# 128 unused bytes a partition ahead of the arena of a transfer-bound attention and mixture-of-experts kernel

## The chip, the cores and the metric

The kernel runs on one core of a Trainium2 chip. The metric is the device time of one execution in microseconds (us), as the median of several executions. The kernel before takes 172.38 us (three executions, 172.25 to 172.53).

## The reference

Everything is float32. Linear attention over 8 batches, 8 heads, 576 positions and 64 channels feeds a soft mixture of 8 experts:

```
kv = einsum('bhsd,bhse->bhde', k, v);  out = einsum('bhsd,bhde->bhse', q, kv)
out = out / sqrt(mean(out*out, -1) + 1e-6) * g_norm
x = out.transpose(0, 2, 1, 3).reshape(4608, 512)
logits = x @ phi                                  # (4608, 32)
d = exp(logits - logits.max(0)); d /= d.sum(0) + 1e-9
slot_input = (d.T @ x).reshape(8, 4, 512)
slot_out[e] = maximum(slot_input[e] @ w1[e], 0) @ w2[e]      # w1 (8, 512, 1024), w2 (8, 1024, 512)
c = exp(logits - logits.max(1)); c /= c.sum(1) + 1e-9
y = c @ slot_out                                  # (4608, 512)
```

## The kernel before, in words

**Memory.** One large tile, `arena`, takes 576 bytes of head (`HEAD` = 144 floats: phi, the norm's gains, and padding) and 160 blocks of 1,024 bytes in each of the 128 partitions. Loads and stores have fixed homes in it, by tables of block numbers (`KV_AT`, `Q_AT`, `W_AT`, `OUT_AT`). `place(at, n)` turns a block number into an access: n floats from 576 + 1,024 * at bytes behind the arena's start. A home is used for attention inputs first, for expert weights later, and for output rows at the end. One weight matrix, ("w1", 7), goes to the tile `xall` instead.

**Addresses.** Tiles are laid one behind another in the order in which the program makes them, each rounded up to a multiple of 32 bytes. The small working tiles of the dictionary `WORK` come first (a name has a number of buffers and a number of floats), then `arena`, `xall` and the constants. Ahead of `WORK` lie 1,152 bytes (1,024 of scratch for the DMA queue of GpSimd and four constants). The buffers of `WORK` take 18,368 bytes, so the arena begins at byte 19,520 of each partition, block 0 of the homes at 20,096, and `xall` at 183,936. 152 bytes a partition are free at the end.

**Work and order.** For each batch, K and V are multiplied into small matrices (`Kv`), whose transposes and products with phi fill `bd`. `products(T)` multiplies a tile of 128 tokens of q by `bd`, which gives attention outputs and raw logits at once. Squares, a row mean, a root and scalings give x and logits, with running sums for the slot inputs. Then 8 experts are computed from the weights as they arrive (`expert_h`, `expert_y`), and `output` makes 12 chunks of the result and stores them. The order is written out by hand. A class `Order` records every instruction, finds what it depends on, and adds the waits, so nearly every instruction is emitted by one line and the profile shows them all as L215.

**Transfers.** Each load is one DMA on SyncE's queue over 128 partitions, one contiguous row of 9,792 to 55,296 bytes in each. Five loads are issued at once, three after batch 0, and the later ones in the order of the program when their homes are free (`loads_behind`, `load_w`). The output is stored in 10 DMAs, two of them on GpSimd's queue, as 608 rows of 6,144 to 24,576 bytes; the last four chunks go as one DMA of 128 rows of 24,576 bytes. In the DMA's access every row starts at an offset that is a multiple of 1,024 bytes from block 0, at the start of `xall`, or, for the very first load (`in_first`, rows of 9,792 bytes), at the start of the arena.

Of the kernel before, what the change touches and what calls it, by code (L numbers as in the profile page):

```python
# [63 lines left out]
HEAD = 144  # L64
SCRATCH = 1024
WORK = {
    "kvT": (1, 256), "sq": (2, 1024), "part": (3, 512), "top": (1, 128), "ms": (3, 16), "r0": (2, 16), "r": (3, 16), "r1": (2, 16),
    "d": (2, 192), "alpha": (2, 1), "cm": (2, 13), "cs": (2, 13),
}
EPS_RMS = 1e-6  # L70
EPS_SUM = 1e-9
# [1052 lines left out]
```

How the kernel before makes its waits and increments, by code:

```python
    def emit(self):  # L204
        nc = self.nc
        counters = {e: nc.alloc_semaphore(f"done_{e}") for e in ENGINES[:4]}
        sems = list(counters.values())
        counts = dict.fromkeys(counters, 0)
        for op in self.ops:
            method, args, kwargs = op.call
            engine = getattr(nc, op.engine)
            *before, last = sorted(op.waits, key=lambda w: w.i) or [None]
            for w in before:
                engine.wait_ge(w.sem, w.value)
            inst = getattr(engine, method)(*args, **kwargs)
            if last is not None:
                inst.wait_op(last.sem, last.value, "sem-ge")
            if op.dma:
                op.sem, op.value = nc.alloc_semaphore(f"dma_{op.i}"), 16
                sems.append(op.sem)
                inst.then_inc(op.sem, 16)
            elif op.signals:
                counts[op.engine] += 1
                op.sem, op.value = counters[op.engine], counts[op.engine]
                inst.then_inc(op.sem, 1)
        *stores, last = [op.sem for op in self.ops if op.dma and not op.signals]
        numbers = sorted(s.num for s in sems)
        assert numbers == list(range(numbers[0], numbers[-1] + 1)) and numbers[-1] == last.num
        for sem in stores:
            nc.sync.wait_ge(sem, 16)
        nc.sync.sem_clear(range(numbers[0], last.num))
        nc.sync.wait_ge(last, 16)
        nc.sync.sem_clear(range(last.num, last.num + 1))
```

## Time and profile before

| | |
|---|---|
| median of three executions | 172.38 us (172.25 to 172.53) |
| the profiled execution's own time | 172.46 us |
| its span, first to last instruction | 171.1 us |
| granted TensorE clock, mean | 0.979 |
| moved by DMA | 71.65 MB, mean 419 GB/s over the span |
| busy: TensorE, ScalarE, VectorE, GpSimd | 148.7, 88.6, 86.5, 59.7 us |

A packet in the views of DMA is one row of a transfer, as the numbers of packets and their bytes show, or a few bytes that signal its end. The DMA share of a stretch is the time that its packets took over 16 engines' time in it; packets are counted where they start, so a short stretch can show over 100%.

### The profile page before, as it was taken

How to read it: one execution, taken by the hardware profiler on the slowest of the kernel's cores; microseconds unless marked ns; L12 is line 12 of the kernel's file. 1: busy time of each engine (PE TensorE's matmuls, PEld its weight loads, DVE VectorE, ACT ScalarE, POOL GpSimd, SP SyncE). 2: the span in 40 equal slices, each digit the busy share in tenths (PEclk: the TensorE clock that was granted, in tenths of full speed). 3: DMA queues.
4: the chain of work that ended last, by engine and by line, in shares of the span. 5: the costliest groups of instructions: out<-in, count | busy, mean ns of one | idle time of the engine just before them, and what ended most of it. 6: DMA issues, size and time to landing. Idle time of an engine off the chain costs nothing.

```text
span 171.1 us, 4194 instructions
## 1 busy us (share of the span) xinstructions
PE 148.7 (87%) x1815; PEld 102.2 (60%) x1815; DVE 86.5 (51%) x183; ACT 88.6 (52%) x230; POOL 59.7 (35%) x73
## 2 busy tenths in 40 slices
PE   7988998999999899999899998689999689989200
PEld 3457987979688787797696672256665333545000
DVE  1111437743677364763936799525887036318300
ACT  2015768786965887668849866113212044418300
POOL 7000347757356665356482589300000004000000
PEclk9999999999999999999999999999999999999965
DMA  5999999999999999899999999999999999999996
GB/s 183 435 463 396 485 405 429 434 421 483 414 409 433 443 465 427 375 431 425 421 433 444 419 412 416 440 427 408 429 425 433 462 414 398 424 428 429 422 445 264
DMA packets 3933, 71.65 MB, mean 419 GB/s; under 512 B 742, under 2 KB 742, under 8 KB 874
## 3 DMA queue, kind: packets, MB, share of 16 engines
q1 hardware_dynamic: 3562, 71.18, 97.6%
q8 instruction: 14, 0.23, 0.5%
q0 software_dynamic: 352, 0.20, 0.4%
q14 instruction: 5, 0.04, 0.1%
HBM read 61.94 MB, written 9.44 MB: 417 GB/s over the span
## 4 chain that ended last, share of the span: by engine, by line
DMA 38%; PE 35%; ACT 10%; DVE 9%; issue 1%; SPq 0%
PE psum L215 35%; DMA arena<-in_t_dram 21%; DMA arena<-in_w_dram 11%; DMA arena<-in_kv_dram 6%; DVE ms L215 3%; ACT sq L215 3%; ACT bd L215 2%; DVE logits L215 2%; ACT xall L215 1%; DVE part L215 1%; ACT arena L215 1%; ACT part L215 1%; DVE r L215 1%; ACT r L215 1%; DVE acc L215 1%
## 5 line engine op out<-in xcount | busy, mean ns | idle before, releaser
L215 PE MATMUL psum<-bd,arena 128*128 128x192 f32 (+1 forms) x320 | 56.5, 336 | 2.6 <-ACT bd L215 1.2
L215 PEld LDWEIGHTS psum<-bd,arena 128*128 128x128 f32 (+1 forms) x320 | 45.5, 179 | 10.1 <-ACT xall L215 3.5
L215 DVE TENSOR_REDUCE ms<-sq 128x16 f32<-128x1024 f32 (+1 forms) x19 | 22.0, 1162 | 28.9 <-ACT sq L215 28.8
L215 POOL TENSOR_TENSOR part<-part,r 128x512 f32<-128x512 f32 x17 | 17.8, 1049 | 49.2 <-DVE r L215 49.2
L215 POOL TENSOR_TENSOR xall<-xall,r 128x512 f32<-128x512 f32 x34 | 34.8, 1045 | 0.0
L215 ACT ACTIVATE sq<-psum 128x512 f32<-128x512 f32 x36 | 21.5, 597 | 10.7 <-PE psum L215 10.6
L215 PEld LDWEIGHTS psum<-arena 128*64 128x64 f32 (+1 forms) x640 | 18.7, 137 | 7.1 <-issue 3.2
L215 PE MATMUL psum<-arena 128*64 128x64 f32 (+1 forms) x640 | 21.3, 226 | 0.6 <-DMA arena<-in_kv_dram 0.4
L215 ACT COPY xall<-psum 128x512 f32<-128x512 f32 x34 | 20.6, 607 | 0.0
L215 ACT COPY part<-psum 128x256 f32<-128x256 f32 (+1 forms) x38 | 13.7, 360 | 10.5 <-DVE part L215 9.3
L215 DVE TENSOR_REDUCE logits<-part 128x64 f32<-128x512 f32 x17 | 17.7, 1043 | 0.0
L215 PE MATMUL psum<-arena,xall 128*32 128x256 f32 x256 | 15.0, 380 | 1.7 <-DMA arena<-in_w_dram 1.7
L215 DVE COPY arena<-psum 128x768 f32<-128x768 f32 (+1 forms) x12 | 10.5, 890 | 6.8 <-PE psum L215 6.8
L215 ACT COPY arena<-psum 128x768 f32<-128x768 f32 (+1 forms) x14 | 10.2, 754 | 7.1 <-PE psum L215 7.1
L215 PE MATMUL psum<-logits,part 32*128 32x384 f32 x96 | 12.7, 527 | 0.6 <-ACT arena L215 0.4
L215 POOL DMA_DIRECT2D out_dram<-arena x2 | 1.2, 590 | 34.2 <-DVE arena L215 34.2
L215 PEld LDWEIGHTS psum<-arena,xall 128*32 128x32 f32 x256 | 8.1, 110 | 8.2 <-issue 2.7
L215 PE MATMUL psum<-arena,sq 128*32 128x256 f32 x224 | 12.7, 379 | 0.2 <-DVE sq L215 0.2
L215 PE MATMUL psum<-xall,d 128*32 128x258 f32 x144 | 10.8, 390 | 1.2 <-ACT d L215 1.2
L215 ACT COPY bd<-psum 64x128 f32<-64x128 f32 (+1 forms) x32 | 9.9, 308 | 2.4 <-PE psum L215 2.2
L215 PEld LDWEIGHTS psum<-arena,sq 128*32 128x32 f32 x224 | 7.2, 110 | 5.1 <-DVE sq L215 0.5
L215 ACT COPY kvT<-psum 128x256 f32<-128x256 f32 (+1 forms) x9 | 3.1, 349 | 12.6 <-PE psum L215 12.6
(81 smaller groups left out, 124.9 us busy)
## 6 DMA issues: line engine op xcount, KB each, us to landing
arena<-in_w_dram SPq DMA_DIRECT2D x4, 4096.0 KB, 24.1
arena<-in_w_dram SPq DMA_DIRECT2D x4, 2048.0 KB, 21.7
arena<-in_t_dram SPq DMA_DIRECT2D x1, 6912.0 KB, 35.9
arena<-in_w_dram SPq DMA_DIRECT2D x2, 3072.0 KB, 23.2
arena<-in_kv_dram SPq DMA_DIRECT2D x2, 2304.0 KB, 19.2
arena<-in_kv_dram SPq DMA_DIRECT2D x1, 4608.0 KB, 40.5
arena<-in_kv_dram SPq DMA_DIRECT2D x1, 3584.0 KB, 30.0
arena<-in_kv_dram SPq DMA_DIRECT2D x1, 3328.0 KB, 26.0
```

What stands on the lines that cost most here:

```text
L215: inst = getattr(engine, method)(*args, **kwargs)
```

## The change

`top` moves behind `r1` in the dictionary that lays out the working tiles, and a tile `spare` of 32 floats that nothing reads or writes comes behind it. `ms`, `r0`, `r` and `r1` begin 512 bytes lower than before and `top` 640 bytes higher. All that comes after `spare`, from `d` on, begins 128 bytes higher: the arena at 19,648, block 0 of the homes at 20,224, `xall` at 184,064. 24 bytes a partition stay free. No instruction, transfer, size, order or wait is changed.

```diff
 WORK = {
-    "kvT": (1, 256), "sq": (2, 1024), "part": (3, 512), "top": (1, 128), "ms": (3, 16), "r0": (2, 16), "r": (3, 16), "r1": (2, 16),
-    "d": (2, 192), "alpha": (2, 1), "cm": (2, 13), "cs": (2, 13),
+    "kvT": (1, 256), "sq": (2, 1024), "part": (3, 512), "ms": (3, 16), "r0": (2, 16), "r": (3, 16), "r1": (2, 16),
+    "top": (1, 128), "spare": (1, 32), "d": (2, 192), "alpha": (2, 1), "cm": (2, 13), "cs": (2, 13),
 }
```

## Rows read from the trace of the kernel before

**Rows 1.** The page: busy tenths of DMA in 40 slices, packets, queues.

```profile
DMA  5999999999999999899999999999999999999996
DMA packets 3933, 71.65 MB, mean 419 GB/s; under 512 B 742, under 2 KB 742, under 8 KB 874
q1 hardware_dynamic: 3562, 71.18, 97.6%
q8 instruction: 14, 0.23, 0.5%
q0 software_dynamic: 352, 0.20, 0.4%
q14 instruction: 5, 0.04, 0.1%
```

**Rows 2.** Busy time by stretch: length, engines, granted clock, DMA share, GB/s.

```profile
0.00:5.00 5.00, 3.94 (x8) 1.70 (x9) 0.73 (x3) 1.28 (x1) 3.02 (x14) 1.00 0.61 219
5.00:165.00 160.00, 144.80 (x1809) 100.54 (x1807) 85.78 (x180) 87.35 (x229) 56.68 (x59) 1.00 1.01 429
165.00:168.50 3.50, 0.00 (x0) 0.00 (x0) 0.00 (x0) 0.00 (x0) 0.00 (x0) 0.50 0.98 421
168.50:171.10 2.60, 0.00 (x0) 0.00 (x0) 0.00 (x0) 0.00 (x0) 0.00 (x0) 0.50 0.40 170
```

**Rows 3.** The chain that ended last, in order of time: start, length, what.

```profile
34.59 35.93 DMA arena<-in_t_dram
...
116.57 18.73 DMA arena<-in_w_dram
...
135.43 1.97 PE psum L215 x32
...
159.58 0.54 DVE arena L215
```

**Rows 4.** DMA issues: size of each, us from issue to landing.

```profile
out_dram<-arena SPq DMA_DIRECT2D x1, 3072.0 KB, 10.9
...
arena<-in_first_dram SPq DMA_DIRECT2D x1, 1224.0 KB, 5.3
```

**Rows 5.** DMA from 3.96 to 4.74 us: rows of the first load alone.

```profile
DMA packets 35, 0.34 MB, mean 439 GB/s; under 512 B 0, under 2 KB 0, under 8 KB 0
q1 hardware_dynamic: 35, 0.34, 103.3%
```

**Rows 6.** DMA from 6.5 to 10 us: rows of 17,408 bytes.

```profile
DMA packets 83, 1.44 MB, mean 413 GB/s; under 512 B 0, under 2 KB 0, under 8 KB 0
q1 hardware_dynamic: 83, 1.44, 96.1%
```

**Rows 7.** DMA from 60 to 65 us: rows of 55,296 bytes.

```profile
DMA packets 41, 2.27 MB, mean 453 GB/s; under 512 B 0, under 2 KB 0, under 8 KB 0
q1 hardware_dynamic: 41, 2.27, 104.8%
```

**Rows 8.** DMA from 164 to 168.5 us: stored rows of 24,576 bytes.

```profile
DMA packets 77, 1.89 MB, mean 421 GB/s; under 512 B 0, under 2 KB 0, under 8 KB 0
q1 hardware_dynamic: 77, 1.89, 97.6%
```

**Rows 9.** DMA from 136 to 141 us: weight rows of 32,768 bytes.

```profile
DMA packets 65, 2.13 MB, mean 426 GB/s; under 512 B 0, under 2 KB 0, under 8 KB 0
q1 hardware_dynamic: 65, 2.13, 98.9%
```

**Rows 10.** Waits of TensorE: engine, for whom, us in total, times, longest.

```profile
PE psum L215 <- DMA arena<-in_w_dram: 1.7, 1, 1.7
PE psum L215 <- DVE top L215: 1.5, 2, 1.0
```

## The prediction

> **What bounds the kernel now.** I read the slices of the page first. The DMA line shows nines from the second slice to the last but one, with a single eight [rows 1]. The table by stretch makes this exact: from 5 to 165 us the 16 DMA engines are covered 1.01 times over at 429 GB/s, still 0.98 from 165 to 168.5 us, where no compute engine works any more, and only the last 2.6 us fall off [rows 2]. The reader should see that TensorE, at 144.8 us of the same 160, is busy too but not what ends the kernel. The chain of waits says the same in another form. It names TensorE often, but its longest pieces are loads of 35.93 and 18.73 us from issue to landing, far more than their bytes need: they stand behind other rows [rows 3]. TensorE then waits 1.7 us for one load of weights [rows 10], and from 135.43 to about 160.1 us runs to the issue of the last store. That store's 3,072 KB (3.146 MB) take 10.9 us to land [rows 4]; at 425 GB/s they need 7.4.
>
> So the time is the sum of what the DMA engines do: the time of a row, and the holes between rows, of which there are none to close.
>
> **What a row costs.** A stretch that holds rows of one size alone gives their mean time: share times 16 times the stretch, over the count. The first load's rows of 9,792 bytes take 1.033 * 12,480 ns / 35 = 368.3 ns [rows 5]. Rows of 17,408 bytes take 0.961 * 56,000 / 83 = 648.4 ns [rows 6]. Rows of 55,296 bytes take 1.048 * 80,000 / 41 = 2,044.9 ns [rows 7]. Stored rows of 24,576 bytes take 0.976 * 72,000 / 77 = 912.6 ns [rows 8]. Weight rows of 32,768 bytes take 0.989 * 80,000 / 65 = 1,217.2 ns [rows 9]. The shares are rounded to 0.1%, which makes these good to 0.2 to 1.0 ns.
>
> From the smallest to the largest a byte costs (2,044.9 - 368.3) / (55,296 - 9,792) = 0.03685 ns. What is left over is a fixed part of each row: 368.3 - 360.8 = 7.5 ns for the first load, 648.4 - 641.4 = 7.0 for the load of 17,408, 912.6 - 905.5 = 7.1 for the store, and 1,217.2 - 1,207.3 = 9.9 for the weights. All packets of rows together number 3,933 - 742 - 19 = 3,172 (without the signals of a few bytes and the instruction fetches) [rows 1], or 198 to an engine. A fixed part of 7.5 ns is 1.5 us of the whole time, 0.9% of it.
>
> **The change, part by part.** It removes, adds and moves no instruction and no DMA, and no wait: the same tiles are written and read in the same order. What it changes is where rows begin. Against a grid of 256 bytes, block 0 of the homes goes from 20,096 = 78 * 256 + 128 to 20,224 = 79 * 256, and with it every home, since blocks are 1,024 bytes; `xall` goes from 183,936 = 718 * 256 + 128 to 184,064 = 719 * 256; the first load's home goes from 64 past a line of the grid to 192 past one. So 3,044 of the 3,172 rows go from the middle of a 256-byte line to its start, and 128 rows go from 64 past one to 192 past it.
>
> If a row that begins and ends in the middle of a line of the grid cost extra, the rows of 17,408 and 24,576 bytes (128 past a line, as the destination of a load and as the source of a store) should stand above the first load's, which begins 64 past a line and covers no more lines of 256 than an aligned row of its size would (39). They stand at 7.0 and 7.1 against 7.5 [rows 5, 6, 8]. One line through sources and destinations and two positions, to half a nanosecond: I take the fixed part as independent of the position, and the effect on each row as 0.
>
> The Trainium skill says otherwise ("DMA: Bandwidth & Descriptors", How a descriptor splits into AXI transactions): a transfer is cut into pieces of 256 bytes that begin on multiples of 256, and one that begins off such a multiple also pays for the unused bytes ahead of its start, in steps of 32 bytes. By it a row that begins 128 past a line has 4 steps too many, and the first load's row 2. At the traced 0.03685 ns a byte that is an estimated 4.7 and 2.4 ns, so the rows of 17,408 and 24,576 bytes should stand 2.4 ns above those of the first load; they stand 0.4 to 0.5 below [rows 5, 6, 8]. The sum by the rule would be 0.9 us less, by the trace 0.
>
> The price of position is not directly shown, since nowhere in this trace does a home begin on a multiple of 256. Its bounds: on the side of a gain, the position can cost no more than the fixed part, 7.5 ns on 198 rows, 1.5 us. On the side of a loss, the fixed parts seen spread from 7.0 to 9.9 ns, so I allow 2.9 ns on 198 rows, 0.6 us. I take 0, by the rows that agree at three kinds of row.
>
> The tiles that compute engines use move as well. TensorE reads `arena`, `xall` and `bd` 128 bytes higher, all by the same step; `ms`, `r0`, `r`, `r1` and `top` change places among themselves. They are written and read by the same instructions with the same sizes, and I cost them at 0. The cover for an error here is the DMA queue, which is full all the time [rows 2]: TensorE's waits for VectorE's `top` are 1.5 us in total [rows 10], and a few tenths more would be hidden behind transfers except between 135.43 and 160 us, where TensorE runs to the last store.
>
> Would a gain come through? The last store is issued at about 160.2 us, needs 7.4 us, and lands after 10.9. The first load, with nothing ahead of it, needs 1.253 MB / 429 GB/s = 2.9 us and lands after 5.3 [rows 4], so about 2.4 us are start and completion, and 10.9 - 7.4 - 2.4 = 1.1 us is the last store's time behind other rows. A saving up to about 1.1 us passes in full; its larger part comes ahead of 135.3 us, where TensorE waits for weights, so the issue moves earlier with it too.
>
> The sum: 172.46 us (span 171.1 and 1.4 around it) + 0 = 172.46 for the profiled execution, which is 0.08 above the median. The median should stay at 172.4.
>
> **The rivals.**
>
> *Every row gets cheaper.* If the 128 bytes between the start of a line and the start of a row are moved or waited for as well, they cost 128 * 0.03685 = 4.7 ns a row now and nothing on an aligned home. On 190 rows an engine (3,044 / 16) that is 0.9 us; 171.5 us. For it speaks that DMA is the only bound, so that any saving counts, and that no aligned home is there to compare with. Against it speaks that the first load does not stand lower. The rule of the Trainium skill named above ("DMA: Bandwidth & Descriptors", How a descriptor splits into AXI transactions) is this rival, if it holds for both sides of a transfer.
>
> *Only stores get cheaper,* if only the side that reads pays for unused bytes: 608 rows, 38 an engine, 4.7 ns each, 0.18 us; 172.2 us, on the edge of what can be measured. Against it: stored rows [rows 8] lie on the line of the loads [rows 6], although only the stores read from a home.
>
> *The weights' excess goes.* The weight rows cost 9.9 ns beyond their bytes, 2.8 more than others [rows 9]. There are 11 loads of weights, so 88 such rows an engine; if that excess came from the position, 0.25 us would go; 172.2 us, and with the stores' 0.18 together 172.0. Against it: the rows of 17,408 and 24,576 bytes have the same position without the excess [rows 6, 8].
>
> *Slower.* The excess of the weight rows shows that something meets some transfers and not others. If the new position, at which every row begins on the same phase of the 256-byte grid, brought it to all rows, each would cost up to 2.9 ns more, 0.6 us on 198 rows: 173.0 us. It decides from 1.7 ns a row (0.34 us over 198). For it: the DMA engines have no spare time to take it. Against it: all homes share one phase already, 128, and stay in step with one another.
>
> *The change doesn't align anything,* if tiles were laid out otherwise than I add them up: 172.4 us, the same as the forecast.
>
> **How the numbers follow.** A difference of 0.2%, 0.34 us, is about what can be told from no change here, the three executions being 0.28 us apart. Forecast (no effect, with the last rival in it) 0.45. Every row cheaper 0.25 (faster). Only stores 0.06 and only the weights' excess 0.04 (both same), the two together 0.06 (faster). Slower 0.14. That makes faster 0.31, same 0.55, slower 0.14. The likeliest case alone would be 172.2 to 172.6. The range takes in the case of 171.5 below and half of the slower case above: 171.4 to 172.8.
>
> **What will show it.** In the changed kernel's trace I would work out the five row times again. The forecast wants 648.4 and 912.6 ns back to half a nanosecond; the first rival wants some 643.7 and 907.9, and 429 GB/s between 5 and 165 us to become 431 to 432; the store rival wants only the 912.6 to fall. The first load's rows, which get no alignment, should not fall in any case, and under the first rival rise by 4.7 ns, since they begin another 128 bytes into their line. If rows keep their time and the kernel still changes, the cause lies in holes between rows or in what meets the weights' rows. The prediction is wrong if the fixed part of a row depends on its start after all, which the trace before could show only through one unaligned case against another.

## The result and the profile after

The changed kernel takes 171.72 us (six executions, 171.63 to 171.91) against 172.38 (six, 172.25 to 172.53). The ratio is 0.9963, with a 95% interval of 0.995 to 0.9976: faster by 0.66 us, 0.37%. Forecast was no change, 172.4 us; the time lies inside the stated range. The profiled execution took 171.91 us with a span of 170.6, so it shows 0.5 us of the gain.

The page of the changed kernel, its slices of DMA and the sum of its packets:

```profile
DMA  5999999999999999999999999999999999999996
DMA packets 3933, 71.65 MB, mean 420 GB/s; under 512 B 742, under 2 KB 742, under 8 KB 874
```

and its busy time by stretch (from and to, length, TensorE, weight loads, VectorE, ScalarE, GpSimd, granted clock, DMA share, GB/s):

```profile
5.00:165.00 160.00, 144.43 (x1809) 100.56 (x1807) 85.82 (x180) 87.29 (x229) 56.61 (x59) 0.98 1.01 430
165.00:168.50 3.50, 0.00 (x0) 0.00 (x0) 0.00 (x0) 0.00 (x0) 0.00 (x0) 0.50 1.01 435
168.50:170.60 2.10, 0.00 (x0) 0.00 (x0) 0.00 (x0) 0.00 (x0) 0.00 (x0) 0.50 0.30 129
```

The same packets and bytes as in [rows 1], and the engines still full to the end as in [rows 2], at 430 GB/s for 429. The eight among the nines is gone. TensorE's granted clock between 5 and 165 us is 0.98 for 1.00, so a faster clock is not where the gain comes from. In the chain of the changed kernel the load of weights that TensorE waits for lands at 116.43 + 18.25 = 134.68 us:

```profile
116.43 18.25 DMA arena<-in_w_dram
134.68 0.14 issue
134.81 1.97 PE psum L215 x32
```

In [rows 3] it landed at 135.30. So 0.62 us are there by the landing of that load. Where they come from is seen in the packets started in two stretches. From 2 to 31 us, the kernel before and the changed one:

```profile
DMA packets 807, 12.22 MB, mean 421 GB/s; under 512 B 80, under 2 KB 80, under 8 KB 80
```

```profile
DMA packets 806, 12.22 MB, mean 421 GB/s; under 512 B 80, under 2 KB 80, under 8 KB 80
```

and from 31 to 143 us, before and changed:

```profile
DMA packets 1983, 48.02 MB, mean 429 GB/s; under 512 B 250, under 2 KB 250, under 8 KB 250
```

```profile
DMA packets 1994, 48.25 MB, mean 431 GB/s; under 512 B 251, under 2 KB 251, under 8 KB 251
```

Nothing is gained in the first 31 us. In the next 112 us, 0.23 MB more get through, which at 429 GB/s is 0.54 us. The rows say why. From 60 to 65 us, rows of 55,296 bytes in the changed kernel:

```profile
DMA packets 40, 2.21 MB, mean 442 GB/s; under 512 B 0, under 2 KB 0, under 8 KB 0
q1 hardware_dynamic: 40, 2.21, 102.0%
```

That is 1.020 * 80,000 / 40 = 2,040.0 ns a row, against 2,044.9 [rows 7]. From 70 to 75 us, rows of 32,768 bytes, before and changed:

```profile
DMA packets 64, 2.10 MB, mean 419 GB/s; under 512 B 0, under 2 KB 0, under 8 KB 0
q1 hardware_dynamic: 64, 2.10, 97.3%
```

```profile
DMA packets 64, 2.10 MB, mean 419 GB/s; under 512 B 0, under 2 KB 0, under 8 KB 0
q1 hardware_dynamic: 64, 2.10, 97.0%
```

1,216.3 and 1,212.5 ns. These are means. The trace also has the time of each packet, and there the excess is no fixed fee: of the 64 rows of this stretch 63 took 1,213 ns in the changed kernel, while before 16 took 1,213 and the other 48 between 1,214 and 1,225. But early rows and stored rows keep their time. In the changed kernel, from 6.5 to 10 us (17,408 bytes) and from 164 to 168.5 us (stores of 24,576 bytes):

```profile
q1 hardware_dynamic: 82, 1.43, 94.9%
```

```profile
q1 hardware_dynamic: 79, 1.94, 100.1%
```

648.1 ns for 648.4 [rows 6], and 912.3 for 912.6 [rows 8]. So the position of a row's start costs less than 0.5 ns in the rows of 17,408 bytes before 10 us and in the stores, and in the two sizes of load shown between 31 and 143 us 3.8 and 4.9 ns a row.

### The profile page after: what moved, and what is told of

Same layout as the page of the kernel before. It is cut to its first block, busy times and chain, and to the rows that moved or that the text cites. A ratio compares the mean times of both kernels' runs of the same rounds, so it can differ in the third digit from the quotient of the medians.

```text
span 170.6 us, 4194 instructions
## 1 busy us (share of the span) xinstructions
PE 148.4 (87%) x1815; PEld 102.3 (60%) x1815; DVE 86.5 (51%) x183; ACT 88.6 (52%) x230; POOL 59.6 (35%) x73
## 4 chain that ended last, share of the span: by engine, by line
PE 51%; DMA 17%; ACT 15%; DVE 9%; issue 1%; SPq 0%
PE psum L215 51%; DMA arena<-in_w_dram 11%; DMA arena<-in_kv_dram 6%; ACT bd L215 4%; ACT sq L215 4%; DVE ms L215 3%; ACT xall L215 2%; DVE logits L215 2%; ACT part L215 1%; DVE part L215 1%; ACT arena L215 1%; ACT r L215 1%; DVE r L215 1%; ACT d L215 1%; DVE acc L215 1%
```

## The experiments

All were timed beside the kernel before (172.39 to 172.41 us; 172.47 and 172.52 beside the two kernels that have one execution each). "Off" means homes that don't begin on a multiple of 256 bytes.

### The two halves of the edit

Only the unused bytes (`spare` in, `top` stays):

```diff
-    "d": (2, 192), "alpha": (2, 1), ...
+    "spare": (1, 32), "d": (2, 192), "alpha": (2, 1), ...
```

> Only the 128 unused bytes; top stays ahead of ms. Theory G (where rows begin against a 256-byte grid): homes on multiples of 256, so all of the change's gain, about 171.7 us, and rows of 32,768 bytes at 1,212.5 ns between 70 and 75 us as in the changed kernel, against 1,216.3 before. Rival T (the small tiles that compute engines use changed places): no gain, 172.4 us.

172.18 us (171.72 to 172.38), ratio 0.9979 [0.9969, 0.9988]. Between 70 and 75 us its rows are as short as the changed kernel's, 0.986 * 80,000 / 65 = 1,213.5 ns:

```profile
q1 hardware_dynamic: 65, 2.13, 98.6%
```

Only the move of `top`:

```diff
-    "top": (1, 128), "spare": (1, 32), "d": (2, 192), ...
+    "top": (1, 128), "d": (2, 192), ...
```

> Only the move of top behind r1, no unused bytes; homes stay 128 past a multiple of 256. Theory G: 172.4 us, rows of 32,768 bytes at about 1,216 ns. Rival T: 171.7 us.

172.36 us (172.25 to 172.43), ratio 0.9995 [0.9986, 1.0003]: no change, and the row time of the kernel before:

```profile
q1 hardware_dynamic: 64, 2.10, 97.3%
```

The rows get shorter with the unused bytes and not with the move of the small tiles, as theory G says. But the time of the first, 0.23 us below the kernel before, is nearer to the middle than to 171.7, so the changed kernel was run again:

> The changed kernel once more, unchanged, beside the three below on one chip. The unused bytes alone gave 172.18 us with single executions from 171.72 to 172.38, the changed kernel 171.72 before. If the position of top and ms matters a little, this gives 171.7 again with little spread; if the aligned kernels simply scatter more from execution to execution, its executions reach from 171.6 to 172.3 as well.

171.86 us (171.67 to 172.11), ratio 0.9969 [0.9957, 0.9981]. All kernels with aligned homes scatter more than those without: their single executions lie between 171.63 and 172.41, those of the full kernels with homes off between 172.22 and 172.62, but for three of the kernel before at up to 173.23. The intervals of this run and of the unused bytes alone overlap, but that doesn't make them equal: eleven executions of the changed kernel in all lie between 171.63 and 172.11, the eleven with the unused bytes alone have their median at 172.18. Neither reading is shown by this run, which stood beside the kernel before on another chip than the unused bytes alone. What decides on `top` is the kernel with the logits ahead of the arena, below: it has `top` in its old place and the whole gain. Why the unused bytes alone gave less stays open.

### Other distances

64 unused bytes instead of 128 (the diff), and 32 (the same line with `"spare": (1, 8)`):

```diff
-    "top": (1, 128), "spare": (1, 32), ...
+    "top": (1, 128), "spare": (1, 16), ...
```

> The changed kernel with 64 unused bytes instead of 128: homes begin 192 past a multiple of 256. Theory G: off the grid is off the grid, no gain, 172.4 us or a little more, rows of 32,768 bytes at about 1,216 ns. Rival S (any other layout draws a new relation between the engines and the transfers, 128 bytes past the line being a bad one): 171.7 to 172.1 us. Rival P (the excess grows with the bytes by which a row begins past the line): more than 172.4, about 172.6 us.

> The changed kernel with 32 unused bytes: homes begin 160 past a multiple of 256 and off multiples of 64 and 128 as well. Theory G: as with 64 bytes, 172.4 us. Rival F (a finer grid, 128 or 64 bytes, counts too, which the homes before were on): slower than before, 172.8 us or more. Rival S: 171.7 to 172.1 us.

172.44 us, ratio 1.0001 [0.9992, 1.001], and 172.40 us, ratio 0.9998 [0.9989, 1.0007]. Neither gains, neither loses. From 71 to 75 us, with 64 bytes and with 32:

```profile
q1 hardware_dynamic: 54, 1.77, 102.7%
```

```profile
q1 hardware_dynamic: 55, 1.80, 104.5%
```

1.027 * 64,000 / 54 = 1,217.2 ns and 1.045 * 64,000 / 55 = 1,216.0. With starts 128, 192 and 160 bytes past a multiple of 256 a row costs about the same, so rivals S, P and F fall: a new layout alone gives nothing, the excess doesn't grow measurably with the distance, and multiples of 64 or 128 bytes give nothing.

A coarser grid, with nothing unused: the tile of the logits (5,504 bytes) is laid ahead of the arena, which puts block 0 at 25,600, a multiple of 1,024.

```diff
+    L = const.tile([P, NT + len(GROUPS) + 1, NS], F32, name="logits")
     arena = const.tile([P, HEAD + ARENA], F32, name="arena")
...
-    L = const.tile([P, NT + len(GROUPS) + 1, NS], F32, name="logits")
```

> The kernel before with the tile of the logits (5,504 bytes) laid ahead of the arena and nothing unused: homes on multiples of 1,024 and not only of 256. Theory G: the same time as the changed kernel, within 0.1 us. Rival K (a coarser grid, 512 or 1,024 bytes, gives more): 171.5 us or less.

171.73 us (171.67 to 172.03), ratio 0.9965 [0.9953, 0.9977]: the changed kernel's time, so 256 is enough. It needs none of the 128 bytes and is no faster. And `top` is where it was before the change, so the gain doesn't need its move.

### Loads or stores

The home of each output chunk is moved 128 bytes on, once in the changed kernel, once in the kernel before.

```diff
+    def out_place(at, n):
+        return arena[:, HEAD + 32 + at * KB : HEAD + 32 + at * KB + n]
...
-        st = place(at, 4 * CT * NS).rearrange("p (a n) -> p a n", a=4)
+        st = out_place(at, 4 * CT * NS).rearrange("p (a n) -> p a n", a=4)
...
```

> The changed kernel with the output rows written and stored 128 bytes further up: loads on multiples of 256, stores off them. Theory L (only loads pay for a start off the grid, as the traces show: the rows of stores took 912.6 ns before): as the changed kernel, within 0.1 us. Rival R (what reads off the grid pays): up to 0.2 us slower than the changed kernel.

> The kernel before with the output rows 128 bytes further up: loads off, stores on multiples of 256. Theory L: 172.4 us, as before, and rows of 32,768 bytes at about 1,216 ns between 70 and 75 us. Rival R: 172.2 us or less.

Aligned loads and stores off: 171.74 us, ratio 0.9967 [0.9955, 0.998]. Loads off and aligned stores: 172.39 us, ratio 0.9995 [0.9986, 1.0005]. Load rows of 32,768 bytes from 70 to 75 us take 0.986 * 80,000 / 65 = 1,213.5 ns in the first and 0.973 * 80,000 / 64 = 1,216.3 in the second. The gain is in the loads.

### Nothing but transfers

Every instruction that is not a DMA is left out of the kernel before and of the changed one; the output is not computed.

```diff
     def add(self, engine, method, args, kwargs):
+        if method != "dma_start":
+            return
```

> The kernel before with every instruction of the compute engines left out: only the 20 loads, the stores of whatever lies in the homes, and the waits among them; the output is not computed. Homes 128 past a multiple of 256. Theory D (transfers off the grid disturb one another, whatever the compute engines do): the excess of the long load rows stays, about 3 ns a row or more, and this kernel is 0.3 to 0.5 us slower than its aligned twin. Rival C (a row off the grid is delayed only where compute engines use the memory at the same time, which would explain why the excess begins only at about 32 us): no excess, and the twins are equal within 0.1 us.

> The same with the changed layout, homes on multiples of 256; again no compute. Theory D: rows of 32,768 bytes at 1,212.5 ns and 0.3 to 0.5 us less than the twin off the grid. Rival C: the same time as the twin.

171.99 us (171.75 to 172.14), ratio to the kernel before 0.9975 [0.9965, 0.9984], and 171.77 us (171.64 to 172.10), 0.9966 [0.9955, 0.9976]. From 70 to 75 us, off and aligned:

```profile
q1 hardware_dynamic: 64, 2.10, 97.4%
```

```profile
q1 hardware_dynamic: 64, 2.10, 97.0%
```

1,217.5 and 1,212.5 ns. The excess is there without any compute engine, so rival C falls: the transfers do it to one another or to themselves.

The difference of the twins, 0.22 us, is less than the 0.3 to 0.5 that theory D wanted, and the traces show where the rest went. What the single rows take beyond the commonest time of their size (1,213 ns for 32,768 bytes, 611 for 16,384), summed from 31 to 143 us, is 0.40 us an engine off the grid and 0.01 on it. Then the aligned twin loses time. From 143.5 to 146.5 us, off and aligned:

```profile
DMA packets 173, 1.24 MB, mean 414 GB/s; under 512 B 88, under 2 KB 88, under 8 KB 100
```

```profile
DMA packets 168, 1.13 MB, mean 376 GB/s; under 512 B 86, under 2 KB 86, under 8 KB 102
```

Between 144 and 146 us, where the last load rows and the first long stores run together, 16 load rows of 16,384 bytes take 676 to 1,149 ns in the aligned twin; in the other none takes over 628 from 140 us on. Summed as above from 143 us on, that is 0.25 us an engine against 0.02, so 0.23 of the 0.39 us are given back. Full kernels with aligned homes have such rows too between 142 and 146 us, 4 to 10 of them over 650 ns in each of the five traces; the full kernels with homes off have 2 each. They may be why aligned kernels scatter more, which is not shown, nor what causes them.

The bare transfers of the changed layout take as long as the changed kernel (171.77 and 171.72 us), but those of the layout before take 0.40 us less than the kernel before. The equal totals don't show that computing is free: between 165 and 168.5 us the DMA share is only 0.67 in the bare aligned kernel, where the changed kernel has 1.01. Without compute the last store on SyncE's queue is issued by about 134.6 us, and not near 160.

### Why only from 31 us on

Transfers alone again, homes off, weights issued ahead of the attention inputs (every DMA is held back with a key in front, 0 for weights, 1 for inputs, 2 for the output, and they are sorted before they are emitted; the diff is cut to that):

```diff
+        held, self.held = self.held, None
+        for _, *call in sorted(held, key=lambda h: h[0]):
+            self.add(*call)
```

> Transfers alone again, homes 128 past a multiple of 256, but the 11 loads of weights are issued ahead of the 9 loads of attention inputs; nothing is computed. It asks why the excess begins only at about 30 us. Theory W (it belongs to the tensors: those read first, up to batch 3, never show it, the later ones and the weights do): weight rows of 16,384 and 32,768 bytes show it from the first microseconds on, at 2 to 5 ns a row, and the rows of 17,408, 18,432 and 26,624 bytes don't show it even late. Rival H (it belongs to the time, or to how the 16 engines' rows have come to lie against one another by then): weight rows before 30 us are as short as on the grid (1,212.5 ns for 32,768 bytes), and the attention rows, now late, are 2 to 5 ns too long.

172.01 us (one execution; the kernel before 172.47 beside it). Weight rows of 32,768 bytes from 24 to 29 us:

```profile
q1 hardware_dynamic: 64, 2.10, 97.0%
```

rows of 17,408 bytes, now from 84 to 87 us:

```profile
q1 hardware_dynamic: 74, 1.29, 100.5%
```

and rows of 26,624 bytes from 98 to 101 us:

```profile
q1 hardware_dynamic: 49, 1.30, 101.1%
```

Early weight rows take 1,212.5 ns although their homes are off: no excess. The rows of 17,408 bytes, 648.4 when they came first [rows 6], take 1.005 * 48,000 / 74 = 651.9, and those of 26,624 take 1.011 * 48,000 / 49 = 990.4. In the kernel before, from 20.5 to 24.5 us, the latter took 0.987 * 64,000 / 64 = 987.0 (64 rows and one packet under 512 bytes):

```profile
DMA packets 65, 1.70 MB, mean 426 GB/s; under 512 B 1, under 2 KB 1, under 8 KB 1
q1 hardware_dynamic: 65, 1.70, 98.7%
```

Theory W falls, rival H holds: the excess belongs to when a row comes, not to which tensor. This rests on one execution and its trace.

Then a pause. The first load of weights waits until all nine input loads have landed.

```diff
+        if op.i == 9:
+            deps.update(range(9))
         self.settle(op, deps)
```

> Transfers alone with homes 128 past a multiple of 256, as in the first of the twins, but the first load of weights is issued only when all nine loads of attention inputs have landed (near 69 us), so that all 16 DMA engines run dry once and start anew; nothing is computed. Theory P (the excess belongs to how the engines' rows have come to lie against one another since they last started from idle): the weight rows behind the pause are clean at first, 1,212.5 ns for 32,768 bytes between 75 and 95 us against 1,217 without the pause, and the excess comes back later. Rival Q (it belongs to the time or to the bytes moved so far): 1,216 to 1,218 ns right behind the pause.

174.94 us (one execution; 172.52 for the kernel before), since the engines run dry between about 68.6 and 70.1 us; with the slower start behind it the time is 3 us above the twin's 171.99. Rows of 32,768 bytes from 75 to 80 and from 84 to 89 us, then rows of 24,576 bytes from 100.5 to 106 and from 115 to 118 us:

```profile
q1 hardware_dynamic: 64, 2.10, 97.0%
```

```profile
q1 hardware_dynamic: 65, 2.13, 98.6%
```

```profile
q1 hardware_dynamic: 96, 2.36, 99.5%
```

```profile
q1 hardware_dynamic: 54, 1.33, 103.0%
```

1,212.5 and 1,213.5 ns, where the twin without a pause had 1,217.5 between 70 and 75 us; then 0.995 * 88,000 / 96 = 912.1 ns, still without excess, and 1.030 * 48,000 / 54 = 915.6 with it. The pause clears it and it comes back, as theory P says.

What brings it on is less clear than that. By the single packets, lengthened rows begin at about 29 us in the twin without a pause, at about 40 with the weights first, and at about 110, 40 us after the new start, behind the pause. But each time, rows of 18,432 or 16,384 bytes had followed on longer ones 2 to 3 us before (at 26.5, 38 and 107 us). So it can be the time since the start, or such a change of the row size after it; no run parts the two.

## Why the prediction was wrong

**What bounds the kernel: right.** The DMA engines are full to the end in both kernels, and shorter rows made a shorter kernel. A gain in the rows came through to the end, as worked out: 0.62 us at the landing of the weights, 0.5 in the span.

**The step that failed: "I take the fixed part as independent of the position, and the effect on each row as 0."** It rested on rows before 10 us and on stores, and for these it was right to 0.3 ns (648.4 to 648.1, 912.6 to 912.3). The first load, which was to rise by 4.7 ns under the first rival, is too uneven for such a reading: from 3.96 to 4.74 us the changed kernel has 32 rows at 95.9%, which is 374.0 ns, and its second run 34 at 100.3%, 368.2, for 368.3 [rows 5]. By the single packets the median row of this load takes 368 ns in all three. Rows before 10 us and stores were no sample of the loads between 31 and 143 us, which are over half of all rows and showed the price in [rows 7, 9]. The line through the rows was drawn with the 55,296 bytes of [rows 7], which held 4.9 ns of it. With 2,040.0 in its place a byte costs (2,040.0 - 648.1) / 37,888 = 0.03674 ns, and the 9.9 ns of the weights [rows 9] become 1,217.2 - 1,203.8 = 13.4, against 648.1 - 639.5 = 8.6 for the early rows. The excess was 4.8 ns, not 2.8. So the term that the sum put at 0 was 3.8 to 4.9 ns on the loads measured in the middle.

**The mis-sized rival.** "The weights' excess goes" was the right mechanism in part: the excess did come from the position. The prediction priced it at 2.8 ns on 88 rows an engine, 0.25 us, and gave it 0.04. It was 3.8 to 4.9 ns on the (1,983 - 250) / 16 = 108 packets an engine between 31 and 143 us, input rows among them, 0.41 to 0.53 us. The single packets, summed from 31 to 143 us as for the twins above, give 0.47 us an engine (1.13 less 0.66). Against this rival stood that rows at the same position had no excess; that argument would have needed the same position at the same time of the kernel.

**"Every row gets cheaper", 171.5 us,** was near in time and wrong in kind: no early row and no stored row got cheaper. The rule of the Trainium skill ("DMA: Bandwidth & Descriptors", How a descriptor splits into AXI transactions) wants 4 steps of 32 bytes on every row that begins 128 past a line and 6 at 192; no run here shows that, neither in the early rows nor in the stores nor between the layouts at 128 and 192 (172.41 and 172.44 us).

**Compute tiles, cost 0: right.** Moving `top` and its neighbours alone gave 172.36 us, and the whole gain comes with them in their old places (171.73 us).

**Luck.** The stated range held the result, but by way of "every row gets cheaper", whose mechanism is not what happened. The forecast itself said no change.

**What stays open.** Which relation between the engines' rows makes the excess is not shown, nor whether time or a change of the row size brings it on; only that it comes under unbroken streaming and that a pause clears it. Why stores never show it isn't either. Of the 0.5 us by which the profiled span got shorter, rows take 0.47 less between 31 and 143 us and 0.07 more after it; the remaining 0.1 us may lie between rows, or in which engine ends last, which was not measured apart.

## What to carry to other kernels

Where the profile shows the DMA engines full from end to end, a small gain (here 0.4%) can lie in addresses: lay out the tiles so that the rows of loads begin on multiples of 256 bytes; putting an existing tile ahead of the arena does it as well as unused bytes. To price a row from a trace, compare rows at the same stage of the kernel: fit the bytes and the fixed part on early rows, and see whether later ones stand above that line. A fixed part that differs between two stages asks for an experiment before it is put at 0.

## What the runs showed of the hardware that was not expected

In the middle of the kernel a load row of 32,768 bytes that begins 128, 160 or 192 bytes past a multiple of 256 takes 3.5 to 5 ns more in the mean than an aligned one (1,216.0 to 1,217.5 ns for 1,212.5), and one of 55,296 bytes 4.9 more; at 36,864 bytes it is 1.8 by the single packets (1,370.1 for 1,368.3). The excess first showed about 28 to 40 us after the engines had started from idle, in each case just after a change to shorter rows. Before that, and for about 40 us behind a gap of 1.5 us in the stream, the same positions cost 1 ns at most. The excess is there with no compute engine at work, and rows of stores don't show it.
